# Attention scores of a fused attention + MoE kernel: the block mask moves into unused rows of the second product's contraction, and a DMA makes the second copy of the high part of k

## The reference, cut to what matters

```python
scores = scale * np.matmul(q, k.transpose(0, 1, 3, 2))      # per head 576 x 576, contraction 64
mask = (pos // 64)[:, None] >= (pos // 64)[None, :]
scores = np.where(mask, scores, -1000000000.0)
scores = scores - np.max(scores, axis=-1, keepdims=True)
attn = np.exp(scores); attn = attn / (np.sum(attn, axis=-1, keepdims=True) + 1e-09)
attn_out = np.matmul(attn, v)                               # then x = attn_out, two MoE layers
```

## Time and profile before

| what | value |
|---|---|
| median of 3 runs | 1209.39 us (1208.06 to 1209.45) |
| profiled execution, its own time | 1211.28 us |
| its span on the core | 1209.3 us |
| attention, first product to last | 13.8 to 259.3 us of the span |
| PE busy, whole span | 1095.4 us (91%) |
| DVE, ACT, POOL busy, whole span | 548.3, 371.3, 522.0 us |

### The profile page before, as it was taken

How to read it: one execution, slowest core, us unless ns; L and a number is a source line. 1 busy time by engine, 2 the same in 40 slices (tenths; PEclk the granted TensorE clock), 3 DMA queues, 4 the chain that set the end, 5 groups by cost and what they waited for, 6 DMA issues and landing times. The chain is left out here.

```text
span 1209.3 us, 18421 instructions
## 1 busy us (share of the span) xinstructions
PE 1095.4 (91%) x6320; PEld 990.8 (82%) x6321; DVE 548.3 (45%) x1130; ACT 371.3 (31%) x898; POOL 522.0 (43%) x264
## 2 busy tenths in 40 slices
PE   4999999989999999999994599797979797989987
PEld 4888888868899898989893598687878787878875
DVE  6887878755323332425145423425252525253341
ACT  3777777755222221213121411111111111111110
POOL 7776777710000202021111337564757666574722
PEclk9999999989999999999996699898989899998989
DMA  8644444426690101010010624353443332533203
GB/s 233 140 99 99 98 98 98 98 69 193 222 382 19 54 0 52 0 52 17 35 52 35 241 92 96 115 113 113 104 119 98 68 114 61 162 64 120 37 1 44
DMA packets 69638, 118.11 MB, mean 98 GB/s; under 512 B 7776, under 2 KB 25312, under 8 KB 69600
## 3 DMA queue, kind: packets, MB, share of 16 engines
q1 hardware_dynamic: 60960, 97.61, 27.2%
q0 software_dynamic: 8640, 20.00, 8.4%
HBM read 81.00 MB, written 36.59 MB: 97 GB/s over the span
## 5 line engine op out<-in xcount | busy, mean ns | idle before, releaser
L1348 PE MATMUL ps_hT<-xT_high,ew_high 128*128 128x256 f32 (+3 forms) x512 | 164.2, 321 | 45.7 <-DVE hT_low L1441 43.8
L782 POOL DMA_INDIRECT expert_rows<-x_rows,slot_idx x36 | 41.1, 1142 | 312.4 <-DVE slot_idx L923 303.3
L1348 PE MATMUL ps_hT<-xT_low,ew_high 128*128 128x256 f32 (+3 forms) x512 | 161.2, 315 | 0.0
L1348 PE MATMUL ps_hT<-xT_high,ew_low 128*128 128x256 f32 (+3 forms) x512 | 160.9, 314 | 0.0
L1348 PEld LDWEIGHTS ps_hT<-xT_high,ew_high 128*128 128x128 f32 x512 | 102.7, 201 | 48.0 <-DVE hT_low L1441 45.8
L1365 PE MATMUL ps_y<-ew_high,hT_high 128*128 128x512 f32 x320 | 129.2, 404 | 1.3 <-DVE hT_low L1441 1.3
L1365 PE MATMUL ps_y<-ew_low,hT_high 128*128 128x512 f32 x320 | 126.8, 396 | 0.0
L1365 PE MATMUL ps_y<-ew_high,hT_low 128*128 128x512 f32 x320 | 126.8, 396 | 0.0
L1403 ACT ACTIVATE hT_high<-ps_hT 128x384 fp32r<-128x384 f32 (+1 forms) x128 | 56.0, 438 | 216.9 <-PE ps_hT L1348 216.4
L1441 DVE SCALAR_TENSOR_TENSOR hT_low<-ps_hT,hT_high 128x384 fp32r<-128x384 f32 (+1 forms) x128 | 60.9, 488 | 135.2 <-ACT hT_high L1403 135.0
L1466 DVE TENSOR_SCALAR y_tile<-ps_y,weight_of 128x512 f32<-128x512 f32 x40 | 30.0, 751 | 178.5 <-PE ps_y L1365 178.5
(11 more groups left out here) (193 smaller groups left out, 2762.8 us busy)
## 6 DMA issues: line engine op xcount, KB each, us to landing
spare<-e_w SPq DMA_DIRECT2D x16, 1024.0 KB, 5.3
w_raw<-e_w SPq DMA_DIRECT2D x16, 1024.0 KB, 7.9
q_raw<-qT SPq DMA_DIRECT2D x36, 288.0 KB, 4.3
k_raw<-kT SPq DMA_DIRECT2D x36, 288.0 KB, 5.4
expert_rows<-zeros SPq DMA_DIRECT2D x8, 1290.0 KB, 14.4
ex_rows<-expert_rows SPq DMA_DIRECT2D x40, 258.0 KB, 4.0
out<-zeros SPq DMA_DIRECT2D x11, 512.0 KB, 10.5
v_raw<-v SPq DMA_DIRECT2D x16, 256.0 KB, 4.9
```

The lines of the kernel that those rows point to most:

```text
L782: nc.gpsimd.indirect_dma_start(out=rows_dram, out_offset=bass.IndirectOffsetOnAxis(ap=slot_idx[:, k, t:t + 1], axis=0), in_=x_rows[:, t, : ...
L1348: mm = nc.tensor.matmul(ps_hT[q % HS][:, 0:rows.stop - rows.start], lhsT[:, c, f * P:(f + 1) * P], rhs[:, c, rows], start=(n == 0), stop=( ...
```

## The change

The three products become two. `q_high` holds q high in both halves of the partitions and `k_parts` k high above k low; `q_rest` holds q low above rows that carry the mask's row pattern, and `k_again` k high above rows with -2^30 at the masked keys. The product of low part with low part is dropped. The mask rows are an input, loaded once at the start by four DMAs issued from POOL (288 KB each). The copy of k high that `k_again` needs is made for each pair by a DMA from SBUF to SBUF, also issued from POOL, between `k_part` and the subtraction for k low; PE waits for it (`k_copied`) at step 0. The subtractions now write 64 partitions, with 1152 elements in each as before.

```diff
@@ block.gpsimd
+            for u in range(2):
+                nc.gpsimd.dma_start(q_rest[u][D:2 * D], masks[0].bitcast(F32R)).then_inc(masks_loaded, 16)
+                nc.gpsimd.dma_start(k_again[u][D:2 * D], masks[1].bitcast(F32R)).then_inc(masks_loaded, 16)
             nc.gpsimd.memset(v_raw[:], 0.0).then_inc(zeroed, 1)
-            nc.gpsimd.memset(mask_raw[:], 0.0).then_inc(mask_filled, 1)
-            ...
@@ cut_qk
                 pool.wait_ge(q_high_ready, n + 1)
-                nc.gpsimd.tensor_tensor(q_split[u][D:2 * D], q_raw[u][D:2 * D], q_split[u][D:2 * D].bitcast(F32),
-                                        ALU.subtract).then_inc(q_cut, 1)
+                nc.gpsimd.tensor_tensor(q_rest[u][0:D], q_raw[u][0:D], q_high[u][0:D].bitcast(F32), ALU.subtract).then_inc(q_cut, 1)
                 pool.wait_ge(k_high_ready, n + 1)
-                pool.wait_ge(q_cut, n + 1)
-                nc.gpsimd.tensor_tensor(k_low[u][:], k_raw[u][:], k_high[u][:].bitcast(F32), ALU.subtract).then_inc(k_cut, 1)
+                pool.sem_inc(waited_pool, 1)
+                nc.gpsimd.dma_start(k_again[u][0:D], k_parts[u][0:D]).then_inc(k_copied, 16)
+                nc.gpsimd.tensor_tensor(k_parts[u][D:2 * D], k_raw[u][D:2 * D], k_parts[u][D:2 * D].bitcast(F32),
+                                        ALU.subtract).then_inc(k_cut, 1)
@@ after the memsets, before the first cut_qk
+            pool.wait_ge(k_high_ready, 1)
+            nc.gpsimd.dma_start(k_again[0][0:D], k_parts[0][0:D]).then_inc(k_copied, 16)
@@ block.vector, pair 0 (q_part and k_part only change the names of what they write)
-            nc.vector.tensor_tensor(k_low[0][:], k_raw[0][:], k_high[0][:].bitcast(F32), ALU.subtract).then_inc(k_cut, 1)
+            nc.vector.tensor_tensor(k_parts[0][D:2 * D], k_raw[0][D:2 * D], k_parts[0][D:2 * D].bitcast(F32), ALU.subtract)\
+                .then_inc(k_cut, 1)
@@ block.scalar
-            nc.scalar.copy(mask_rows[:], mask_raw[:, 0:P]).then_inc(masks_ready, 1)
-            nc.scalar.copy(mask_keys[:], mask_raw[:, P:P + BLOCK]).then_inc(masks_ready, 1)
@@ product
                     pe.wait_ge(q_cut, n + 1)
+                    pe.wait_ge(k_copied, 16 * (n + 1))
...
-                    nc.tensor.matmul(out, lhsT, k_high[u][:, j, a:a + step], start=True, stop=False)
-                    if i < FULL:
-                        nc.tensor.matmul(scores[0:R, bank[t], W - BLOCK:W], mask_rows[:], mask_keys[:], start=False, stop=False)
-                    mm = nc.tensor.matmul(out, lhsT, k_low[u][:, j, a:a + step], start=False, stop=True)
+                    nc.tensor.matmul(out, q_high[u][:, j, rows_of], k_parts[u][:, j, a:a + step], start=True, stop=False)
+                    mm = nc.tensor.matmul(out, q_rest[u][:, j, rows_of], k_again[u][:, j, a:a + step], start=False, stop=True)
@@ before the first product
-            pe.wait_ge(masks_ready, 2)
+            pe.wait_ge(masks_loaded, 64)
@@ host
+    for i in range(S // (2 * block)):
+        masks[0, i, :, place // block == 2 * i] = 1
+        masks[1, i, :, place // block == 2 * i + 1] = -2.0 ** 30
```

More of the change, by code:

```diff
@@ L13, with attention @@
 META = 4
-def attention(nc, qT, kT, v, identity, xT, prefetch, prefetched):
+def attention(nc, qT, kT, v, identity, masks, xT, prefetch, prefetched):
     _, _, D, S = qT.shape
@@ L30, in attention @@
     HALF = S // 2
-    MASKED = -1e9
     SCALE = D ** -0.5
@@ L68, in attention @@
         v_raw = sb("v_raw", [P, TILES, 2 * D])
-        q_split = [sb(f"q_split{u}", [P, 2, S], F32R) for u in range(2)]
-        k_high = [sb(f"k_high{u}", [P, 2, S], F32R) for u in range(2)]
-        k_low = [sb(f"k_low{u}", [P, 2, S], F32R) for u in range(2)]
+        q_high = [sb(f"q_high{u}", [P, 2, S], F32R) for u in range(2)]
+        q_rest = [sb(f"q_rest{u}", [P, 2, S], F32R) for u in range(2)]
+        k_parts = [sb(f"k_parts{u}", [P, 2, S], F32R) for u in range(2)]
+        k_again = [sb(f"k_again{u}", [P, 2, S], F32R) for u in range(2)]
         v_high = [sb(f"v_high{u}", [P, TILES, 2, 2 * D], F32R) for u in range(2)]
@@ L97, in attention @@
         waited_pe = sem("waited_pe")
+        waited_pool = sem("waited_pool")
         qk_loaded = [sem(f"qk_loaded{u}") for u in range(2)]
@@ L108, in attention @@
         scores_ready = sem("scores_ready")
-        mask_filled = sem("mask_filled")
-        masks_ready = sem("masks_ready")
+        masks_loaded = sem("masks_loaded")
+        k_copied = sem("k_copied")
         max_found = sem("max_found")
@@ L241, in _ @@
                     cut_v(2 * m + u, u, False)
+            pool.wait_ge(k_copied, 16 * (LAST + 1))
         @block.vector
@@ L272, in q_part @@
                 dve.wait_ge(q_scaled, n + 1)
-                nc.vector.tensor_copy(q_split[u][:], q_raw[u][:]).then_inc(q_high_ready, 1)
+                nc.vector.tensor_copy(q_high[u][:], q_raw[u][:]).then_inc(q_high_ready, 1)
             def k_part(half, u):
                 dve.wait_ge(qk_loaded[u], 64 * (half + 1))
-                nc.vector.tensor_copy(k_high[u][:], k_raw[u][:]).then_inc(k_high_ready, 1)
+                nc.vector.tensor_copy(k_parts[u][:], k_raw[u][:]).then_inc(k_high_ready, 1)
             def emit(b, first):
@@ L310, in _ @@
             dve.wait_ge(k_high_ready, 1)
[L311 removed]
+            nc.vector.tensor_tensor(k_parts[0][D:2 * D], k_raw[0][D:2 * D], k_parts[0][D:2 * D].bitcast(F32), ALU.subtract)\
+                .then_inc(k_cut, 1)
             dve.wait_ge(q_high_ready, 1)
[L313 to L314 removed]
+            nc.vector.tensor_tensor(q_rest[0][0:D], q_raw[0][0:D], q_high[0][0:D].bitcast(F32), ALU.subtract).then_inc(q_cut, 1)
             batches(dve, emit)
@@ L389, in product @@
                     pe.wait_ge(q_cut, n + 1)
+                    pe.wait_ge(k_copied, 16 * (n + 1))
                 if not (fresh and before[t] < 0):
                     pe.wait_ge(exp_done, STEPS * n + before[t] + 1)
-                lhsT = q_split[u][:, j, i * P:i * P + R]
+                rows_of = slice(i * P, i * P + R)
                 step = HALF if W > 512 else W
@@ L1486, in _, with bass_attention_moe @@
             through(dve, stretch)
-def bass_attention_moe(nc, qT, kT, v, w1, w2, w3T, w_out, w_gate_noise, noise, e_w1, e_w2, const_in, C, out):
+def bass_attention_moe(nc, qT, kT, v, w1, w2, w3T, w_out, w_gate_noise, noise, e_w1, e_w2, const_in, masks, C, out):
     P = 128
@@ L1528, in bass_attention_moe @@
                          (consts[:], const_in), (counts[:], const_in[:, C["start"]:C["start"] + E])]
-            attention(nc, qT, kT, v, const_in[:, C["ident"]:C["ident"] + P], xT, prefetch, prefetched)
+            attention(nc, qT, kT, v, const_in[:, C["ident"]:C["ident"] + P], masks, xT, prefetch, prefetched)
             w1_high, w1_low, w2_high, w2_low = (part(moe, name, DC, F) for name in ("w1_high", "w1_low", "w2_high", "w2_low"))
@@ L1577 @@
     const[:, C["earlier"]:] = np.tril(np.ones((E + 1, E)), -1).reshape(-1)
+    block = 64
+    place = np.arange(S)
+    masks = np.zeros((2, D, 2, S), np.float32)
+    for i in range(S // (2 * block)):
+        masks[0, i, :, place // block == 2 * i] = 1
+        masks[1, i, :, place // block == 2 * i + 1] = -2.0 ** 30
     arrays = {
@@ L1591 @@
         "const_in": const,
+        "masks": masks,
     }
```

7 lines of the change are left out of this document (removed).

## The result

The change made the kernel slower: 1215.49 us in the median of 6 runs (1212.6 to 1215.67), against 1209.42 us for the kernel before in 6 runs of the same session (1207.51 to 1209.98). The ratio is 1.0047, 95% interval 1.0034 to 1.0060, some 6 us. The forecast was 1205.0 us and its range ended at 1214. The profiled execution took 1215.64 us, its span was 1213.8 us.

The account below looks back on a forecast made before the run. PE was taken to set the pace of attention's pairs. Pairs -9.9 and start +5.5 make -4.4 us on the profiled 1211.28, 1206.9; with the median 1.9 lower, 1205.0 us, range 1199 to 1214.

Parts of the forecast that it names:

- Mask price, 0.11 us, and six of eight that count: PE's steady pairs: each mask product costs 0.11 us, six of eight count, 0.66 us a pair, 9.9 us over 15 pairs.
- the lock: SBUF port of DVE and POOL: a DVE cast can block POOL's DMA issue; about 1 us more for the first issue.
- The rival in which the pairs don't follow PE: Steady pairs: DVE's chain sets them and the masks are worth nothing; 1214.9 us, chance 0.10.
- POOL's issue and gap, d = 1.26: POOL's order in each pair: issuing the copy plus its gap takes d = 1.26 us, bounds 0.3 and 2.69.
- The rival with a long d: POOL bounds every pair: at d = 2.69 a pair takes 15.25 us, total 1223; chance 0.07 beyond 1215.
- d is free up to 1.64 us for q: Loop from `q_part` to `q_part`, 12.56 + d against a 14.20 us pair: d costs nothing up to 1.64 us.
- The rival in which POOL is the bound: Loop `q_part` to `q_part` sets pairs from d = 1.64; chance 0.12 between 1205 and 1215 us, 0.07 beyond.
- The start, +5.5: Before steady pairs: pair 1's later q, 4.3 us, plus d once, 1.26, say 5.5 us; bounds 1 and 11.
- The first loads were costed at 2.8 us late: Start: mask loads halve the first q and k set's rate, so DVE finishes pair 0 at 16.5, not 13.8.
- The first product, forecast at 17.7: PE, pair 0: waits for the copy, 3.9 us later than 13.82; before 15 or after 20 would be wrong.
- The copy lands in time: Steady pairs: lands 2.7 to 4.3 us from issue, before step 0 needs it; late-copy rival 1209.5 us, chance 0.06.
- The sum: Whole kernel: -9.9 from the pairs and +5.5 from the start make -4.4 us, predicted time 1205.0 us.

Follow-up runs that it names:

- experiment 1: The changed kernel without DVE's `row_den` (1e-9 left out of the denominator); 1207.15 us, ratio 0.9976 to the kernel before.
- experiment 3: The changed kernel without the copy of k high and PE's wait for it, the second product reading `k_parts` (result not the reference's); 1204.90 us.
- experiment 9: The changed kernel with copies issued by SP, mask rows cleared by ACT and four rows loaded, no `row_den`, weight prefetch one pair later; 1202.82 us.
- experiment 10: The kernel of experiment 9 with `row_den` kept, so nothing of the computation is left out; 1204.93 us, ratio 0.9965 to the kernel before.
- experiment 8: The changed kernel with ACT clearing the mask rows and v low, POOL loading only the four rows that are not zero; 1209.70 us.
- experiment 7: The kernel before plus four unused loads of 288 KB issued by POOL ahead of its memsets; 1215.45 us, ratio 1.0049.
- experiment 2: The kernel before without DVE's `row_den`; 1208.29 us, ratio 0.9995.
- experiment 4: The kernel before with an unused copy of k high issued by POOL each pair and PE's wait for it from pair 1 on; 1211.79 us.
- experiment 5: The changed kernel with POOL clearing the mask rows by four memsets and loading only the four rows that aren't zero; 1215.62 us.
- experiment 6: The changed kernel with the prefetch of weights issued one pair later; 1213.48 us, ratio 1.0043 to the kernel before.

## Why the prediction was wrong

- **Mask price, 0.11 us, and six of eight that count: right.** The price is 0.11 us in experiment 1 with 512 columns, and at the turn of a pair PE waits 0.20 us longer (the transposes start 0.50 us after the last product, at 137.18 and 137.68 in the changed kernel, where 0.30 stood before). Where the lock is out of the way the pair takes 14.16 to 14.21 us (experiments 1, 3, 9, 10), against the 14.20 worked out. With `row_den` kept (3, 10) that is 0.70 us below the mean pair of before, 14.90, where 0.66 was forecast. The rival in which the pairs don't follow PE falls with it.
- **POOL's issue and gap, d = 1.26: right in size.** From `k_part`'s end (145.17) to the subtraction (146.36) are 1.19 us, where 0.08 stood before: d = 1.1. The wait for v, which the prediction left 0.05 us of slack, did not bind: v was finished at 137.88, and PE's `values` began at 137.99, behind its transposes. The rival with a long d did not come: the copy's 17 issues took 0.51 to 0.57 us, the first of them too (15.73 to 16.24), though DVE's cast of q ran until 16.10. One issue was longer, the last mask load of experiment 8: 1.04 us (8.83 to 9.87), beside DVE's tensor_scalar, which ended at 9.78.
- **"d is free up to 1.64 us for q": the step that failed in the pairs.** It took DVE's `q_part` for the first that can be late behind POOL's scaling. That is so by semaphores. By the shared port it is `row_den`, which runs before `q_part`. Its slack in the trace was 132.12 - 130.96 = 1.16 us. The change takes 0.66 of that by the shorter pair and 1.1 by d, 1.76 in all, so 0.6 us were missing, and 14.20 + 0.6 = 14.8 is the pair that was measured (14.74). The rival in which POOL is the bound had the right loop and the wrong last link, so that its threshold of d = 1.64 was 1.1 us too high: with the lock d is free up to 1.16 - 0.66 = 0.5. The lock had been weighed only as DVE holding up POOL's issues; here POOL held up DVE. Cost: some 0.54 x 14 = 7.6 us.
- **The start, +5.5: undersized, the second step that failed.** In the two traces pair 1 starts 9.0 us later. The first loads were costed at 2.8 us late; it was 5.8, and 6.3 in experiment 7 (14.70 us, where experiments 2 and 4 had 8.40). The estimate does not follow from its own premise: at 240 GB/s the 1.18 MB of the first set take 4.9 us, and at half the rate 4.9 more, not 2.8. DVE and everything behind it moved by what was measured. POOL's issues, costed at 1.26 us each, took 0.5 to 0.7; they were off the path. The first product, forecast at 17.7, came at 20.59, beyond the 20 that the prediction had set as a sign of being wrong. It waited for the copy, which was the right wait.
- **"The copy lands in time": right in the steady pairs, wrong in pair 1.** It landed after 3.1 us in the median, within the 2.7 to 4.3 of the rows of before. In pair 1 it shared the engines with the prefetch (a load of 2 MB among it, 12.3 us to landing) and took 7.
- **The sum.** In the median the loads alone cost 6.6 us (experiment 7) and the pairs gave back about 0.16 x 14 = 2.2, not 9.9. With the copy's waits, 1.5 at pair 0 and 1.2 at pair 1, that makes 7.1, against the 6 measured; the medians of the runs are no surer than that.

**What the clock did.** The last pair with its tail took 26.7 us in the changed kernel, where it took 25.1 before and 25.2 in experiment 8, which has the changed kernel's pairs. In the changed kernel PE's granted clock was 0.50 from 263 to 266 us; in the other two it was 1.00 until the end of attention. Experiment 10 shows the same, a tail of 26.1 us with the clock at 0.50 from 251 to 254. So these 1.5 us belong to the execution, not to the two products. In pairs 0 and 1 the changed kernel ran at the lower clock as well, and the kernel before did not: the window of 27.0 to 37.4 us, before and then after (length, busy time and count of PE, PEld, DVE, ACT and POOL, then PE's clock).

```profile
27.00:37.40 10.40, 10.40 (x73) 9.19 (x71) 9.32 (x18) 7.84 (x25) 7.68 (x4) 1.00 0.89 230
```
```profile
27.00:37.40 10.40, 9.10 (x38) 7.40 (x37) 7.27 (x16) 6.96 (x20) 8.38 (x7) 0.51 1.09 328
```

In the 3 us ahead of it, 24 to 27, PE had been busy for 0.9 us. How much of the time that pairs 0 and 1 took is due to this, and how much to the copy's wait, was not separated.

What stays open: pair 0 takes 11.25 us in the trace of before and 13.20 in those of experiments 2 and 7, which don't touch it. There PE works more slowly for longer: in experiment 2 the transposes at 20.5 us took 0.87 us in place of 0.52, at a granted clock shown as 1.00. So up to 2 of the 9.0 us by which pair 1 starts later may belong to the execution and not to the change. Nor was it settled why the stages behind attention took 3 us less in the profiled execution; the spread of the runs (3 us) is as large. That `k_part` is held by the port is read from its ends alone; no run takes that hold away.

## What to carry to other kernels

When work moves on GpSimd, list not only who waits for it by semaphore but every VectorE instruction that a GpSimd instruction can hold by the shared port, however small, and read its slack; one pair of the trace in which it is already long is the warning. A constant that is mostly zeros is cheaper cleared by an idle engine than loaded, when the loads stand beside the first data of the kernel; the engine must not be one that holds the port of the first instruction (experiment 5). And a copy that replaces arithmetic should be issued from a queue whose next work can wait: in the steady pairs the same DMA cost nothing from SyncE (14.20 us a pair with it, 14.21 with no copy). Beside large loads it came late from either queue, 6.9 us after its issue from GpSimd and 9.7 from SyncE.

## What the runs showed of the hardware

- A tensor_scalar on VectorE between SBUF buffers of 128x10 elements took 0.17 us alone and up to 2.06 us under a GpSimd tensor_tensor (pair 1 of experiment 6), always until 0.02 to 0.03 us after its end; one of 128x1152 took 7.63 us in place of 0.76 under a chain of memsets. The tensor_tensor and reduce operations of VectorE that read PSUM kept their lengths (0.28 us at 128x128) beside the same GpSimd work.
- A cast of 128x1152 took 0.75 us alone, 1.37 us beside GpSimd's subtraction in the steady pairs and 2.40 in pair 0 (`k_part`, 23.92 us, changed kernel). It ended 0.61 to 0.63 us after the subtraction each time.
- The issue of a direct DMA from GpSimd took 0.51 to 0.75 us, once 1.04, and started 0.3 to 0.6 us after the instruction that released it (15.43 to 15.73, 145.17 to 145.75).
- PE's granted clock fell to 0.50 for some 10 us in pairs 0 and 1 and for some 3 us in the tail of attention, in some executions and not in others with the same pairs. In the tail that cost 1.5 us.
